# Attention and two expert layers on one core: VectorE's small steps in another form, expert rows placed earlier in a tile

## The reference, cut to what matters

```python
scores = (z @ z.T) / S                     # per batch, S = 2496, 4 batches, d_qk = 64
x = u * (maximum(scores, 0)**2 @ v)        # 9984 tokens, D = 256

# layer 1: only tokens with x @ w_skip > 0
e = argmax(x @ w_gate);  g = softmax(x @ w_gate)[e]        # 8 experts
x = x + g * (maximum(x @ w1[e], 0) @ w2[e])                # F = 1024; other tokens keep x

# layer 2: every token
e = argmax(x @ w_gate2 + bias[modality]);  g = softmax(...)[e]
out = g * (maximum(x @ w1b[e], 0) @ w2b[e])
```

## Time and profile before

| | us |
|---|---|
| median of 3 runs | 1569.56 (1567.95 to 1569.83) |
| the profiled execution | 1574.07 |
| its span | 1572.3 |
| PE busy in the span | 1514.6 |
| DVE busy | 1013.3 |
| ACT busy | 776.4 |
| POOL busy | 466.1 |

### The profile page before, as it was taken

The page is one execution under the profiler, slowest core; times in us unless marked ns, Lnnn a source line. Parts: engine busy times, 40 slices in busy tenths (PEclk is TensorE's granted clock), DMA queues, the critical chain, the costliest instruction groups (busy, mean ns, idle before and its releaser), DMA issues.

```text
span 1572.3 us, 38375 instructions
## 1 busy us (share of the span) xinstructions
PE 1514.6 (96%) x13409; PEld 1379.5 (88%) x13409; DVE 1013.3 (64%) x2382; ACT 776.4 (49%) x1463; POOL 466.1 (30%) x434
## 2 busy tenths in 40 slices
PE   8999999999999999998999999998999999999996
PEld 6878887788778887887988988988999999999996
DVE  7989977888788989876566666654333333333332
ACT  6677766676677767663444434443322322322321
POOL 4133412343133324222444444443211111111111
PEclk9999999999999999999999999998999999999998
DMA  5311031203002022112433333321311111111110
GB/s 114 95 42 49 27 109 33 63 31 99 27 29 62 27 82 80 30 40 92 139 126 114 127 129 126 99 79 46 101 48 41 48 54 41 48 48 41 48 48 26
DMA packets 60108, 106.41 MB, mean 68 GB/s; under 512 B 18183, under 2 KB 32018, under 8 KB 59980
## 3 DMA queue, kind: packets, MB, share of 16 engines
q1 hardware_dynamic: 41788, 46.66, 10.8%
q0 software_dynamic: 18192, 58.13, 10.8%
HBM read 75.35 MB, written 30.94 MB: 68 GB/s over the span
## 4 chain that ended last, share of the span: by engine, by line
PE 78%; DMA 6%; DVE 4%; issue 4%; POOL 3%; ACT 2%; POOLq 0%; DVEq 0%; SPq 0%; ACTq 0%
PE pO L1238 29%; PE pO L1430 18%; PE pS L1446 18%; PE pS L1227 8%; DMA token_rows<-xrow,dest 4%; POOL VL L466 2%; DMA raw<-in_v_dram 2%; PE pT L1378 1%; PE pT L1286 1%; DVE take L1110 1%; DMA A<-in_w2t_dram 1%; PE pO L1247 1%; DVE take L1109 1%; PE pM L1296 1%; PE pO L1360 1%
## 5 line engine op out<-in xcount | busy, mean ns | idle before, releaser
L1430 PE MATMUL pO<-ZH,VH 128*128 x2016 | 402.5, 288 | 2.3 <-issue 2.3
L1446 PE MATMUL pS<-VL,AH 128*128 128x256 f32 (+1 forms) x2016 | 370.3, 284 | 21.5 <-DVE AL L1159 21.5
L785 ACT ACTIVATE AH<-pO 128x512 fp32r<-128x512 f32 x252 | 151.0, 599 | 401.7 <-PE pO L1430 401.4
L1446 PEld LDWEIGHTS pS<-VL,AH 128*128 128x128 f32 x2016 | 311.8, 190 | 25.3 <-DVE AL L1159 25.2
L1430 PEld LDWEIGHTS pO<-ZH,VH 128*128 128x128 f32 x2016 | 328.3, 192 | 4.0 <-issue 4.0
L961 DVE TENSOR_TENSOR AL<-A,AH 128x512 fp32r<-128x512 f32 (+1 forms) x400 | 305.1, 763 | 13.7
L1238 PE MATMUL pO<-AH,VH 64*128 64x512 f32 (+1 forms) x1520 | 301.0, 386 | 3.7 <-DVE xT L870 2.3
L1238 PE MATMUL pO<-AH,VL 64*128 64x512 f32 (+1 forms) x1520 | 298.7, 383 | 0.0
L1238 PE MATMUL pO<-AL,VH 64*128 64x512 f32 (+1 forms) x1520 | 298.3, 382 | 0.0
L1159 DVE SCALAR_TENSOR_TENSOR AL<-pO,AH 128x512 fp32r<-128x512 f32 x252 | 172.7, 691 | 187.9 <-ACT AH L785 184.1
L659 ACT ACTIVATE R<-pS 128x512 f32<-128x512 f32 (+1 forms) x400 | 213.6, 587 | 157.5 <-PE pS L1227 148.4
(11 more groups left out here) (194 smaller groups left out, 1584.4 us busy)
## 6 DMA issues: line engine op xcount, KB each, us to landing
raw<-in_w_dram POOLq DMA_DIRECT2D x22, 1024.0 KB, 7.1
xin<-token_rows SPq DMA_DIRECT2D x65, 268.0 KB
uT<-in_u_dram SPq DMA_DIRECT2D x16, 512.0 KB
A<-in_w2t_dram POOLq DMA_DIRECT2D x8, 1024.0 KB
raw<-in_v_dram SPq DMA_DIRECT2D x4, 1152.0 KB, 5.9
raw<-in_v_dram SPq DMA_DIRECT2D x4, 768.0 KB, 7.6
raw<-in_z_dram SPq DMA_DIRECT2D x8, 368.0 KB
token_rows<-pad_row SPq DMA_DIRECT2D x10, 268.0 KB
```

The source lines that it names most:

```text
L785: s_.activation(hH[p], pO[:, p * 512:(p + 1) * 512], ACT.Relu).then_inc(q.h_hi, 1)
L1430: last = t_.matmul(pO[:, p * 512 + fi * TT:p * 512 + (fi + 1) * TT], w[h][:, kd, f * P:(f + 1) * P], x[:, ds(par, 1), kd, :].rearrange("p ...
L1446: last = t_.matmul(pS[s][:, 0:width], a[p][:, fi * TT + s * P:fi * TT + (s + 1) * P], w[h][:, f, 0:width], start=(f == 0 and n == 0), stop ...
```

## The change

Five edits:

1. A helper `two(out, a, b, op)` computes `(a * 1.0) op b` as one scalar-tensor-tensor instruction. It takes the place of most of DVE's tensor-tensor steps, among them the low part AL in attention. Small copies become `max(a, a)` in the same form. The four small tensor-scalar steps of routing become the same form, with the constant tensors `one_f` and `big_f` as second operand where one is needed. The cast AH (L959) stays a cast.
2. In stage 0 DVE's work on the rows of the tile before is cut in three, and moved ahead: `best_logit` before `h_low(0)`, `pick_expert` after it, `place_tile` after `h_low(2)`.
3. ACT's `exp_tile` moves ahead of `h_high(2)` and `stage_rows` between `h_high(2)` and `keep_x`; PE's `prefix_x2` moves from the end of the tile to the place after `layer2(0)`.
4. ACT instead of DVE makes the high parts of the first five pieces of V.
5. POOL's `split_low` makes each piece in one instruction of 128x1024 instead of two of 128x512.

```diff
@@ POOL, split_low
-                    for half in range(2):
-                        w = half_piece(n, half)
-                        ins = g_.tensor_tensor(wl[w], raw[w], wh[w].bitcast(F32), ALU.subtract)
-                    ins.then_inc(wl_ready, 1)
+                    g_.tensor_tensor(wl, raw, wh.bitcast(F32), ALU.subtract).then_inc(wl_ready, 1)
@@ ACT, attention
             z_high(0, 0)
+            v_high(0, 0)
             z_high(0, 1)
...
+                    if g == 0 and p < VU // 2 - 1:
+                        v_high(0, p + 1)
@@ ACT, a tile
                             take_x(t + 1, (t + 1) % 2)
+                            rows_before(exp_tile)
                             h_high(2)
+                            rows_before(stage_rows)
                             keep_x(t + 1, (t + 1) % 2)
                             start(1)
-                            if ph == 0:
-                                with act.If(t > 0):
-                                    exp_tile(t)
                             h_high(3)
                             start(2)
-                            if ph == 0:
-                                with act.If(t > 0):
-                                    stage_rows(t)
                             start(3)
@@ DVE
+            def two(out_, a, b, op):
+
+                return v_.scalar_tensor_tensor(out=out_, in0=a, scalar=1.0, in1=b, op0=ALU.mult, op1=op)
...
-                v_.tensor_copy(xrow[:, :, TOK:TOK + 3], meta[:, ds(4 * idx, 4), :]).then_inc(meta_ready, 1)
+                two(xrow[:, :, TOK:TOK + 3], meta[:, 4 * idx:4 * idx + 4, :], meta[:, 4 * idx:4 * idx + 4, :], ALU.max).then_inc(meta_ready, 1)
...
-                    v_.tensor_tensor(AL[k % NBUF][:, 0:n], A[k % NA][:, 0:n], AH[k % NBUF][:, 0:n].bitcast(F32),
-                                     ALU.subtract).then_inc(al_ready, 1)
-
-            V_AT = {0: (1,), 1: (2, 3), 2: (4,), 5: (5, 6), 6: (7,), 7: (8,), 8: (9,)}
+                    two(AL[k % NBUF][:, 0:n], A[k % NA][:, 0:n], AH[k % NBUF][:, 0:n].bitcast(F32), ALU.subtract).then_inc(al_ready, 1)
+
+            V_AT = {4: (5,), 5: (6,), 6: (7,), 7: (8,), 8: (9,)}
...
-                    step(v_.tensor_scalar(take[:, 0:T, 0], x2a[:, :, TOK], float(N), None, ALU.is_lt))
-                    step(v_.tensor_scalar(take[:, 0:T, 1], take[:, 0:T, 0], -float(BIG), float(BIG), ALU.mult, ALU.add))
...
+                    v_.scalar_tensor_tensor(out=take[:, 0:T, 0], in0=x2a[:, :, TOK], scalar=float(N), in1=one_f[:, 0:T], op0=ALU.is_lt, op1=ALU.mult)
...
+                    step(v_.scalar_tensor_tensor(out=take[:, 0:T, 1], in0=take[:, 0:T, 0], scalar=-float(BIG), in1=big_f[:, 0:T], op0=ALU.mult, op1=ALU.add))
@@ DVE, a tile
+                            rows_before(best_logit)
                             h_low(0)
+                            rows_before(pick_expert)
                             h_low(1)
                             xt_low(t + 1, (t + 1) % 2)
                             h_low(2)
-                            if ph == 0:
-                                with dve.If(t > 0):
-                                    pick_expert(t)
+                            rows_before(place_tile)
                             h_low(3)
...
-                            if ph == 0:
-                                with dve.If(t > 0):
-                                    place_tile(t)
@@ PE, a tile
                             layer2(0)
+                            last_tile(prefix_x2)
                             layer1(3)
                             layer2(1)
                             layer2(2)
                             layer2(3)
-                            last_tile(prefix_x2)
```

More of the change, by code:

```diff
@@ L788, in start, with rows_before @@
                                     ahead((piece,))
+                            def rows_before(part):
+                                if ph == 0:
+                                    with act.If(t > 0):
+                                        part(t)
                             h_high(0)
@@ new lines, in best_logit, with pick_expert @@
+                    step(two(eq[:, 0:T, 1, :], lg[:, 0:T, 1, :], mxb, ALU.is_equal))
+                    two(eq[:, 0:T, 1, :], eq[:, 0:T, 1, :], rev[:, None, :].to_broadcast([P, T, E]), ALU.mult).then_inc(q.step, 1)
+                def pick_expert(idx):
+                    step = stepper(STEPS * idx + 3)
+                    dve.wait_ge(q.step, STEPS * idx + 3)
+                    v_.scalar_tensor_tensor(out=take[:, 0:T, 0], in0=x2a[:, :, TOK], scalar=float(N), in1=one_f[:, 0:T], op0=ALU.is_lt, op1=ALU.mult)
@@ L1116, in pick_expert @@
                     step(v_.tensor_reduce(pick[:, 0:T, 1], eq[:, 0:T, 1, :], AX.X, ALU.max))
-                    step(v_.tensor_tensor(eq[:, 0:T, 1, :], eq[:, 0:T, 1, :], pick[:, 0:T, 1:2].to_broadcast([P, T, E]), ALU.is_equal))
-                    v_.tensor_tensor(oh[:, 0:T, E:GR], eq[:, 0:T, 1, :], take[:, 0:T, 0:1].to_broadcast([P, T, E]), ALU.mult).then_inc(q.onehot, 1)
+                    step(two(eq[:, 0:T, 1, :], eq[:, 0:T, 1, :], pick[:, 0:T, 1:2].to_broadcast([P, T, E]), ALU.is_equal))
@@ L1120, in place_tile @@
+                    step(v_.scalar_tensor_tensor(out=take[:, 0:T, 1], in0=take[:, 0:T, 0], scalar=-float(BIG), in1=big_f[:, 0:T], op0=ALU.mult, op1=ALU.add))
+                    two(oh[:, 0:T, E:GR], eq[:, 0:T, 1, :], take[:, 0:T, 0:1].to_broadcast([P, T, E]), ALU.mult).then_inc(q.onehot, 1)
                 def place_tile(idx):
[L1121 to L1126 removed]
@@ L1128, in place_tile @@
-                    T = SUB
+                    step = stepper(STEPS * idx + 6)
                     dve.wait_ge(q.exp, idx)
                     step(v_.tensor_reduce(den[:, 0:T, 1], ex[:, 0:T, 1, :], AX.X, ALU.add))
-                    step(v_.tensor_scalar(den[:, 0:T, 1], den[:, 0:T, 1], 1e-9, None, ALU.add))
+                    step(v_.scalar_tensor_tensor(out=den[:, 0:T, 1], in0=den[:, 0:T, 1], scalar=1e-9, in1=den[:, 0:T, 1], op0=ALU.add, op1=ALU.max))
                     dve.wait_ge(q.staged, idx + 1)
-                    v_.reciprocal(x2s[:, :, GATE], den[:, 0:T, 1]).then_inc(q.step, 1)
@@ L1139, in place_tile @@
+                    step(two(rank[:, 0:T, 0:E], rank[:, 0:T, 0:E], oh[:, 0:T, E:GR], ALU.mult))
+                    two(base[:, E:GR], prefix[:, T, E:GR], base[:, E:GR], ALU.add).then_inc(q.base, 1)
                     step(v_.tensor_reduce(dest_f[:, 0:T], rank[:, 0:T, 0:E], AX.X, ALU.add))
-                    v_.tensor_tensor(dest[:, 0:T], dest_f[:, 0:T], take[:, 0:T, 1], ALU.add).then_inc(q.dest, 1)
+                    two(dest[:, 0:T], dest_f[:, 0:T], take[:, 0:T, 1], ALU.add).then_inc(q.dest, 1)
@@ L1160, in h_low, with rows_before @@
                                                         in1=hH[p].bitcast(F32), op0=ALU.max, op1=ALU.subtract).then_inc(q.h_split, 1)
+                            def rows_before(*parts):
+                                if ph == 0:
+                                    with dve.If(t > 0):
+                                        for part in parts:
+                                            part(t)
+                            rows_before(best_logit)
                             h_low(0)
+                            rows_before(pick_expert)
                             h_low(1)
```

69 lines of the change are left out of this document (34 added, 35 removed).

## The result

The changed kernel has a median of 1575.14 us in 12 runs (1570.73 to 1579.07), the kernel before 1569.48 us in 12 runs on the same chip (1567.08 to 1572.33). The ratio is 1.0036, with a 95% interval of 1.0024 to 1.0049: slower by 5.7 us, where 1597 us had been forecast. The direction was right, the size was not.

A forecast was written before the change was run, and what follows sets the result against it. PE was taken as the bound, busy 1514.6 of 1572.3 us. Terms −24.9 + 54 − 3.5 + 1.5 = +27.1 on 1574.07 gave 1601.2, less 4.5 a forecast of 1597 us; 8-in-10 range 1553 to 1614, own range 1580 to 1614.

The forecast's parts named there:

- What comes: Stage 0: the wait for `stored`, moved ahead of the last quarter of h, stalls PE and lowers its clock, +54 us.
- The debt: Per expert, T being its first tile's start: PE waits from T + 23.2 to T + 28.9, 5.7 us, seven times, 40 us.
- Its split: Expert's first tile: held steps let `h_low(3)` through near T + 16.6, stalling PE 5.7 us; second tile's stall some 0.2.
- The clock: Stage 0: a half-clock stretch follows each long stall, taken as 2.0 us each, 14 us together.
- What goes: Stage 0: PE's 21.5 us of stalls and 3.4 us of half-clock loss disappear, −24.9 us.
- The end of stage 0: Border to stage 1: `dest` comes about 5.5 us earlier and PE's filler about 1.3 sooner, −3.5 us.
- Attention: Attention: DVE stands before V's second half with two splits of A fewer done, bounds 0 and +3, taken as +1.5 us.
- The new form: Scalar-tensor-tensor on two SBUF operands: taken as no difference, from the nearest row's 692 ns against 693.
- rival C: Attention: the new form is slow on two SBUF operands, 214 us more on DVE, 1706 us; chance 0.05.
- A: Stage 0: the old stalls go and none comes, −26.9 us, 1543 us; chance 0.17.
- B: Stage 0: landing or POOL 2 to 4 us sooner, stalls 2.5 us, −2.4 us in all, 1567 us; chance 0.14.
- seven waits of 5 to 6 us: Sign in the profile after: PE waits seven times, 5 to 6 us each, for the low part of h.

The follow-up runs named there:

- experiment 10: Changed kernel with `place_tile` back behind `h_low(3)` and `stage_rows` back behind `h_high(3)`, POOL's order as changed: 1549.83 us, 0.9871 of the kernel before.
- experiment 3: Changed kernel with POOL's low parts again in two instructions of 512 columns: 1585.53 us, 1.0092 of the kernel before.
- experiment 6: Changed kernel with POOL's row writes ahead of the weight requests and `place_tile` behind `h_low(3)`: 1544.78 us, 0.9838 of the kernel before.
- experiment 1: Changed kernel with all moved row steps back in their old places; new forms, long pieces and V's casts on ACT kept: 1571.98 us, 1.0004 of before.

## Why the prediction was wrong

**The step that failed** is the size of the term "What comes", +54 us: stalls of 5.7 us per expert and 2.0 for the clock. Its mechanism held: a wait for `stored` moved ahead of the last quarter, a debt shared between two tiles, the loss in stage 0 only, gone when the two steps go back (experiment 10). It measured 39.6 us in place of 54. Its numbers were, per expert:

- *The debt*, 5.7 forecast, 4.4 measured in the expert shown, and 27.0 us of pauses in all seven in place of 40. The landing came at T + 25.3, not T + 26.4: the pieces ended at T + 14.9 instead of 15.4, and the second write landed after 6.3 us instead of 6.9. `h_low(3)` ended with PE going on at T + 27.8, not T + 28.9, and was due at T + 23.4.
- *Its split.* I let three small steps be held and PE wait for all of it in the first tile. In five experts of seven `den` slipped past; `h_low(3)` came at T + 13.2, not T + 16.6, and the debt was paid in two pauses.
- *The clock*, 2.0 forecast on top of each debt. Not every pause has a slow stretch behind it. Behind a first pause of 2.3 us the stretch is part of the debt and adds nothing (801.4, 1006.2); behind a second pause (859.4) and behind the first ones of 4.55 and 4.2 us (920.9, 1050.6) it comes on top. Only where the debt is paid whole and late, as in experiment 3, does it come on top seven times: of its 34.1 us 3.4 stand at the start and 4.8 inside the pauses, so (34.1 − 8.2) / 2 = 13 us, near the 14 forecast. There the mechanism and the clock term were right, and the pauses of 4.4 to 5.1 a microsecond too short.

In all 29.4 of pauses (29.7 less 0.3 at the start; one of 2.24 us at 753.6, in the first tiles of all, the forecast had not named) and 6 × 1.7 = 10.2 of clock make 39.6 in place of 54: −14.4.

**The other terms.** *What goes*, −24.9: met as far as it went, but the stretch of 6.8 us at half clock at the start of stage 0 was left out. The tiles of before held 5.8 us of it, which the changed kernel does not have: −2.9. *The end of stage 0*, −3.5: measured −6.3. `dest` came 6 us sooner relative to the last tile's end, as reasoned, but before also ran 6.8 us between the stages at half clock, and this loss went too. *Attention*, +1.5: measured −1.8, near the 1.7 us of the slow stretch at 305.0, which the profile of before has and that of the changed kernel has not; no run shows what the moved casts cost. *Stage 1*, 0: measured −1.4, near the half of the 3.4 us at half clock with which stage 1 began before. Together the sum was 25.9 us too high on the executed times (1601.2 against 1575.27); the terms above make 24.8 of it, and 1.1 stays open. The profile of before stood 4.5 above its median, that of the changed kernel at its own; taking 4.5 off for both gave back 4.4 by luck, so 21.6 remained at the medians. The forecast's own range was added up too narrowly: its extremes sum to +8.6 and +48.1, not to +10 and +44.

**The new form**: right. The median of the low part of A is 693 ns as before; rival C is refuted, and the sentence of the Trainium skill ("Vector Engine (DVE) Microarchitecture Reference", Points that are easy to get wrong) that this form halves throughput with two non-bf16 SBUF sources does not hold in this kernel, on 400 instructions.

**The rivals.** A (no stalls, 1543) is what experiment 10 makes of the change, at 1549.8, and experiment 6 at 1544.8: its price was about right, its condition not met. B (half of each, 1567) had the landing 2 to 4 us sooner; it was 1.1 us sooner, and the time lies between B and the forecast. Of the signs named, these came: PE's waits for the low part of h sum to more than 21.5 us (29.2), nothing changed before 720 us, no 128x2 step over 3 us, pauses in the first tile where small steps are held, a shorter border, and, by a hair, a clock share below 0.97 between 720 and 1083 us (0.967, and 0.972 before). These did not: seven waits of 5 to 6 us (13, up to 4.6), ACT idle for 7 to 9 us (up to 5.0).

## What to carry to other kernels

A step that waits for a transfer costs by what is queued behind it: with 32.6 us of waiting behind the last operand of PE (experiment 10) the kernel was 26 us faster than with 24.6 us of waiting ahead of it. Before moving such a step earlier, issue its transfer earlier: here two row writes in front of two weight requests were worth 0.5% by themselves. With `place_tile` moved back as well the kernel took 1.6% less time than before, of which the two steps put back alone gave 1.3% (experiment 10). When a forecast stacks waits, work out each instruction's start against the start of what would hold it, and give a spread where they are hundredths of a microsecond apart.

## What the runs showed of the hardware

- A DVE step with two SBUF operands that started beside a POOL subtraction ended with it, as scalar-tensor-tensor and as tensor-tensor: 128x16 elements took 2.27 us instead of 0.17 beside a piece of 2.42, and 1.16 beside one of 1.31 (experiment 3). The Trainium skill ("SBUF — State Buffer", Who interferes with whom) speaks of one instruction's length. The trace agrees for the changed kernel's steps, but not everywhere: in experiment 10 a two-operand step on 128x2, which started at 894.16, ahead of two pieces and beside a weight request of POOL, lasted through both, 5.23 us, and in experiment 1 the step at 792.67, which started within the first of two pieces, ended with the second (791.44 + 4.78 = 796.22), 3.59 us later. What decides between one piece and two no run shows: `rank` at 838.93 also started within the first of a pair that ran without a break, and ended with that first.
- POOL's subtraction of 128x1024 took 2.35 to 2.42 us, two of 128x512 2.54: the longer form saves 0.1 to 0.2 us per piece, which in the old order of steps (experiment 1) does not show in the time.
- A pause lowers the clock in some cases only. Those of 2.3 us were followed by 3.4 us at a granted clock of 0.50 in some cases (801.4) and not in others (843.9). Of the pauses of 3.7 to 5.1 us in the tiles of all twelve profiles, 29 in number, each had such a stretch, of 3.4 or 6.8 us, beginning within the pause or at most 1.1 us behind it.
- A row write behind two weight requests in POOL's queue was visible 6.3 us after its start (5.9 to 6.8 over the seven experts), one ahead of them, in experiment 6, 2.4 us after (842.25 to 844.64; 2.3 to 2.6 over the seven):

```profile
842.25 0.98 POOL L577 DMA_INDIRECT token_rows<-xrow,dest  x1 [0.30 <-issue]
```

```profile
844.64 0.64 ACT L757 COPY xrow<-xrow 128x536 f32<-128x536 f32 x1 [1.79 <-DMA token_rows<-xrow,dest]
```
